# A chunked retention kernel with two matrix stages: 64-column state products, later weight splits, a second buffer and a new order of the first loads

## What is computed

```
scores = q @ k^T / 8 ; ret = scores * gamma_h^(i-j) for i >= j, else 0      8 batches, 8 heads, 576 positions, 64 wide
x  = (ret @ v), heads side by side                                          4608 tokens x 512
y  = max(x @ w1, x @ w2, x @ w3) @ w_out                                    512 -> 768 -> 512
a  = y @ u1 ; b = y @ u2 ; out = ((a * b) @ u3) @ u_out                     512 -> 1024 -> 1024 -> 512
```

## Time and profile before

| | us |
|---|---|
| median of 3 runs | 1279.63 |
| lowest, highest | 1277.74, 1281.57 |
| profiled execution | 1278.5 |
| its span in the trace | 1276.7 |
| TensorE busy | 1245.4 (98%) |
| mean granted clock of TensorE | 0.996 of 2.4 GHz |

### The profile page before, as it was taken

One profiled execution on the slowest core, in us unless ns is written; L12 is line 12 of the kernel. 1 busy time (PEld: TensorE's weight loads), 2 busy tenths in 40 slices (PEclk: granted clock), 3 DMA queues, 4 the chain that ended last, 5 costly groups with the idle time before them and its releaser, 6 DMA issues.

```text
span 1276.7 us, 20538 instructions
## 1 busy us (share of the span) xinstructions
PE 1245.4 (98%) x8032; PEld 1223.4 (96%) x8032; DVE 784.2 (61%) x1194; ACT 458.6 (36%) x707; POOL 443.0 (35%) x248
## 2 busy tenths in 40 slices
PE   7999998999999999999999999999999999799999
PEld 6999998999999999999899999999999999699998
DVE  6677755864646465559688677454545356647763
ACT  2122214432323232425455444242324234345442
POOL 4366436520202010043598571202021116525640
PEclk9999999999999999999999999999999999899999
DMA  9999865121212121043556441313223152444441
GB/s 379 309 363 298 278 212 180 62 76 49 75 50 75 50 75 44 31 138 120 180 185 213 151 145 60 106 50 100 74 94 105 51 181 83 142 155 149 155 149 69
DMA packets 82929, 174.37 MB, mean 137 GB/s; under 512 B 8976, under 2 KB 57488, under 8 KB 82832
## 3 DMA queue, kind: packets, MB, share of 16 engines
q1 hardware_dynamic: 82832, 173.05, 39.0%
HBM read 109.58 MB, written 63.44 MB: 136 GB/s over the span
## 4 chain that ended last, share of the span: by engine, by line
PE 46%; DVE 2%; issue 2%; DMA 1%; ACT 1%; SPq 0%; DVEq 0%; ACTq 0%
PE ps L965 15%; PE ps L967 15%; PE ps L966 15%; DMA gd<-h 1%; DVE clo L716 1%; DVE wlo L716 1%; ACT chi L642 0%; DVE h L804 0%; DVE h L851 0%; ACT w L706 0%; DVE h L857 0%; SPq L400 0%; DVE s L851 0%; DVE h L831 0%; DVE h L811 0%
## 5 line engine op out<-in xcount | busy, mean ns | idle before, releaser
L965 PE MATMUL ps<-chi,whi 128*128 128x384 f32 x2016 | 678.0, 336 | 20.5 <-DVE wlo L716 9.5
L966 PE MATMUL ps<-clo,whi 128*128 128x384 f32 x2016 | 676.1, 335 | 0.0
L967 PE MATMUL ps<-chi,wlo 128*128 128x384 f32 x2016 | 676.0, 335 | 0.0
L517 POOL TENSOR_TENSOR raw<-raw,raw 128x768 f32<-128x768 f32 (+2 forms) x96 | 261.4, 2743 | 594.9 <-DMA raw<-xd 207.8
L965 PEld LDWEIGHTS ps<-chi,whi 128*128 128x128 f32 x2016 | 379.7, 188 | 25.4 <-issue 11.6
L966 PEld LDWEIGHTS ps<-clo,whi 128*128 128x128 f32 x2016 | 380.0, 188 | 0.0
L967 PEld LDWEIGHTS ps<-chi,wlo 128*128 128x128 f32 x2016 | 379.8, 188 | 0.0
L716 DVE TENSOR_TENSOR clo<-raw,chi 128x768 fp32r<-128x768 f32 (+2 forms) x168 | 258.1, 1543 | 33.0 <-ACT chi L642 32.8
L642 ACT CAST chi<-raw 128x768 fp32r<-128x768 f32 (+2 forms) x168 | 180.1, 1081 | 89.7 <-PE ps L967 58.5
L706 ACT COPY w<-ps 128x384 f32<-128x384 f32 x126 | 60.5, 480 | 245.9 <-PE ps L967 244.5
L692 ACT COPY u<-ps 128x384 f32<-128x384 f32 x126 | 60.7, 481 | 169.5 <-PE ps L967 168.0
(11 more groups left out here) (41 smaller groups left out, 911.1 us busy)
## 6 DMA issues: line engine op xcount, KB each, us to landing
qks<-qk SPq DMA_DIRECT2D x32, 576.0 KB, 6.1
vks<-vk SPq DMA_DIRECT2D x32, 576.0 KB, 5.6
gd<-h SPq DMA_DIRECT2D x96, 192.0 KB, 1.9
raw<-gd SPq DMA_DIRECT2D x24, 768.0 KB, 6.4
hd<-h SPq DMA_DIRECT2D x72, 192.0 KB, 1.9
raw<-hd SPq DMA_DIRECT2D x24, 576.0 KB, 5.2
raw<-xd SPq DMA_DIRECT2D x24, 384.0 KB, 5.5
x2d<-h SPq DMA_DIRECT2D x48, 192.0 KB, 2.6
```

Of the source, the lines that this page charges most:

```text
L517: return nc.gpsimd.tensor_tensor(out_, a, b, op)
L965: nc.tensor.matmul(to, w1, x1, start=(start and k == 0), stop=False, skip_group_check=True)
L966: nc.tensor.matmul(to, w1, x2, start=False, stop=False, skip_group_check=True)
L967: last = nc.tensor.matmul(to, w2, x1, start=False, stop=(k == KH[st] - 1), skip_group_check=True)
```

## The change

It makes four edits.

- `sum_state` computes, per chunk, two products of 64 weight columns by 64 moving columns, one for each head, each into its own half of the partitions, in place of one of 128 by 128.
- Part 1 of every weight split moves: on ScalarE from after the w copy of iteration W_SPLIT_AT to before the w copy of the next iteration; on VectorE from after "21" of the next iteration to its end, just ahead of part 0 of the following weight. Weight 20, the second of stage O, is split one iteration earlier (113 in place of 114), and the first token block of stage O is split by ScalarE at the end of iteration 112 and by VectorE at the start of 113.
- In stage C a second buffer holds the block of pos 6 of every odd tile, so that its load goes out with the other three.
- The first loads go out in the order qk 0, vtab, vk 0, two heads of dec, qk 1, qtab, vk 1, the other six heads of dec.

```diff
@@ -101,13 +101,13 @@
          ("next", "p4"): [5], ("next", "p3"): [6]}
-HI_IO = {("end", "s"): [0], ("end", "u"): [1], ("end", "p3"): [2], ("end", "p2"): [3],
+HI_IO = {("prev", "w"): [0], ("end", "u"): [1], ("end", "p3"): [2], ("end", "p2"): [3],
          ("next", "p5"): [4], ("next", "p3"): [5, 6]}
...
          ("next", "12"): [5], ("next", "11"): [6]}
-LO_IO = {("end", "21"): [0], ("end", "12"): [1], ("end", "11"): [2, 3], ("next", "22"): [4],
+LO_IO = {("end", "start"): [0], ("end", "12"): [1], ("end", "11"): [2, 3], ("next", "22"): [4],
          ("next", "11"): [5, 6]}
@@ -115,6 +115,8 @@
         table = ci if tau == I * TILES else io if tau == O * TILES else std
+        if tau and it == last_of(tau - 1) - 1:
+            out += [(tau, pos) for pos in table.get(("prev", point), [])]
         if tau and it == last_of(tau - 1):
@@ -136,7 +138,7 @@
 W_SUM_AT = {2: 0, 3: 1, 4: 2, 5: 3, 6: 4, 7: 5, 8: 6, 9: 50, 10: 52, 11: 57, 12: 59, 13: 61, 14: 66, 15: 67, 16: 68,
-            17: 69, 18: 70, 19: 110, 20: 113}
+            17: 69, 18: 70, 19: 110, 20: 112}
 W_SPLIT_AT = {wi: it + (wi >= FIRST_W[C]) for wi, it in W_SUM_AT.items()}
@@ -206,13 +208,13 @@
 
-        raw_at = [[i * KH[st] * N * 4 for i in range(7)] for st in range(3)]
+        raw_at = [[i * KH[st] * N * 4 for i in range(8 if st == C else 7)] for st in range(3)]
         raw_at.append([0, 173056, 12288, 6144, 137216, 179200, 187392])
...
             kh = KH[st]
-            raw.append([at(f"raw{st}_{i}", [P, kh, N], f32, raw_at[st][i]) for i in range(7)])
+            raw.append([at(f"raw{st}_{i}", [P, kh, N], f32, raw_at[st][i]) for i in range(len(raw_at[st]))])
             size = 2 * kh * N * 4
@@ -275,7 +277,7 @@
         vk_loaded = [sem(f"vk_loaded{i}") for i in range(4)]
-        dec_loaded = sem("dec_loaded")
+        dec_loaded = [sem(f"dec_loaded{i}") for i in range(2)]
         vtab_loaded = sem("vtab_loaded")
@@ -322,6 +324,8 @@
         def raw_block(tau, pos):
+            if pos == 6 and tau // TILES == C and tau % 2:
+                return raw[C][7]
             return raw[tau // TILES][pos]
@@ -420,7 +424,7 @@
                 for pos in (0, 3, 6, 2):
-                    if pos != 6 or t == 0 or st in (B, I):
+                    if pos != 6 or t == 0 or st != O:
                         load_raw_block(tau, pos)
@@ -428,12 +432,13 @@
             load_qk(0)
-            sp.dma_start(dec[:, :, :], decay).then_inc(dec_loaded, 16)
+            sp.dma_start(vtab[:, :, :], vdecay).then_inc(vtab_loaded, 16)
             load_vk(0)
-            sp.dma_start(vtab[:, :, :], vdecay).then_inc(vtab_loaded, 16)
+            sp.dma_start(dec[:, 0:2, :], decay[:, 0:2, :]).then_inc(dec_loaded[0], 16)
+            load_qk(1)
             sp.dma_start(qtab[:, :, :], qdecay).then_inc(qtab_loaded, 16)
-            load_qk(1)
             load_vk(1)
+            sp.dma_start(dec[:, 2:HEADS, :], decay[:, 2:HEADS, :]).then_inc(dec_loaded[1], 16)
             load_u3(0)
@@ -504,7 +509,7 @@
                     load_raw(I * TILES)
-                if two_parts:
+                if two_parts and tau // TILES == O:
                     load_raw_rest(tau)
@@ -694,6 +699,9 @@
                 for wi in range(2, NW):
+                    if W_SPLIT_AT.get(wi) == it - 1:
+                        split_weight(wi, 1)
+                for wi in range(2, NW):
                     if W_SPLIT_AT.get(wi) == it:
@@ -705,9 +713,6 @@
                 splits(it, "w")
-                for wi in range(2, NW):
-                    if W_SPLIT_AT.get(wi) == it:
-                        split_weight(wi, 1)
 
@@ -718,8 +723,8 @@
                 dve.wait_ge(scored, n + 1)
-                if n == 0:
-                    dve.wait_ge(dec_loaded, 16)
+                if n < 2:
+                    dve.wait_ge(dec_loaded[n], 16)
                 if n >= 2:
@@ -737,7 +742,7 @@
                         own = slice(h * DH, h * DH + DH)
-                        new = ps[own, S_STATE, c * P + h * DH:c * P + h * DH + DH]
+                        new = ps[own, S_STATE, c * DH:(c + 1) * DH]
                         if c == 0:
@@ -817,9 +822,6 @@
                 splits(it, "21")
-                for wi in range(2, NW):
-                    if W_SPLIT_AT.get(wi) == it - 1:
-                        split_weight(wi, 1)
                 if g >= 0:
@@ -887,9 +892,12 @@
                 for c in range(NC):
-                    last = nc.tensor.matmul(ps[:, S_STATE, c * P:(c + 1) * P],
-                                            vks[n % 4][:, K_AT + c * P:K_AT + (c + 1) * P], vdec[:, c, :],
-                                            start=(c == 0), stop=(c == NC - 1), skip_group_check=True)
+                    for h in range(2):
+                        own = slice(h * DH, h * DH + DH)
+                        keys = K_AT + c * P + h * DH
+                        last = nc.tensor.matmul(ps[own, S_STATE, c * DH:(c + 1) * DH],
+                                                vks[n % 4][:, keys:keys + DH], vdec[:, c, own],
+                                                start=(c == 0), stop=(c == NC - 1), skip_group_check=True)
                 last.then_inc(state_summed, 1)
```

## The result

The changed kernel takes 1259.37 us (median of 4 runs, 1256.64 to 1261.09), the kernel before beside it 1279.14 (1277.74 to 1281.57). The ratio is 0.9841, with a 95% interval of 0.9818 to 0.9865: faster by 20 us. The forecast was 1249.4 with a range of 1243 to 1263; the sign and the range held, and the middle was 10 us too low. The profiled execution took 1258.94 us with a span of 1257.2.

What follows compares the result with a forecast made beforehand. TensorE, busy for 98% of the span, was taken to bound the kernel. 1278.5 - 16.8 - 2.0 + 0.6 + 1.5 - 2.0 - 10.4 = 1249.4 us, with a range of 1243 to 1263.

Steps and rivals of the forecast that it cites:

- State sums: First stage: eight pairs of narrow products take 0.44 us against 0.89; 0.56 us saved a step, -16.8 us over 30 steps.
- The pause: First stage: the 0.09 us pause where full-width products give way to half-width ones stays, but moves ahead of the state sum.
- The cover: First stage: with steps at 5.2 us, VectorE, GpSimd and DMA still keep up, so nothing reaches TensorE; costed at nothing.
- First loads: Start of the kernel: vtab and qk 1 land sooner, so the scores of pair 2 come at 16.3: -2.0 us (-3.5 to 0).
- Second parts, stages B and I: Later weight splits: P6's wait in B goes but sum22 comes late, +0.6 us; in I sum22 is delayed, +1.5 us.
- Second parts, stage C: Later tile changes of stage C: reordering VectorE's splits leaves their sum the same, so nothing expected (-3 to +3).
- Second buffer: Stage C, first tile change: GpSimd's chain moves up by 2.8 us, leaving 0.7 of 2.7 us of waits: -2.0 us (-3 to -1).
- Stage O: Start of stage O: 9.5 us of waits go, 1.9 come, the clock stays up saving about 4: net -10.4 us (-12 to -5).
- issue-bound sums: Rival, first stage: issue and not columns limits the sums, so 3.6 of the 16.8 us are left: 1262.6; chance 0.13.
- The stall of stage O only moves, half won: Rival, stage O: VectorE's list slips 2 us, P6 waits 2 to 3, clock falls; 6 us less won: 1255.4; chance 0.18.
- The serial halves: Rival, first stage: a sum's halves do not run side by side, sixteen products take 1.76 us: 1289.0, slower; chance 0.03.

Runs made afterwards that it cites:

- e1: The kernel before with only the state sums changed to sixteen products of 64 moving columns, loads in the old order: 1264.07 us, ratio 0.9876.
- c2: The changed kernel with the first loads back in the old order: 1256.85 us, ratio 0.9820.
- e3: The kernel before with only the second buffer for the block of pos 6 of stage C: 1273.34 us in a single run.
- e4: The kernel before with block sums of weight 20 and stage O's first token block each an iteration earlier, second parts in old places: 1270.53 us, ratio 0.9932.
- a1: The changed kernel with both engines' second weight parts back at their old places: 1254.01 us, ratio 0.9817.
- b1: a1 with sum22 ahead of the token split of pos 2 in stages C and O from the second tile on: 1249.62 us, ratio 0.9786.
- e2: The kernel before with only the second weight parts at their new places and weight 20's block sums an iteration earlier: 1275.91 us, ratio 0.997.
- a2: The changed kernel with the two loops of a state sum exchanged, halves outer: 1267.21 us in a single run.
- a3: The changed kernel with each state sum made twice, 32 products instead of 16: 1273.43 us in a single run.
- c3: The changed kernel with the first token block of stage O back at its old place: 1259.2 us (two runs).
- c4: The changed kernel without the second buffer of stage C: 1262.03 us.

## Why the prediction was right, and where it was off

- **State sums**: the mechanism was right and a size was off. I had eight pairs of 0.055 = 0.44 us; they take 0.52, which is 8 x 0.058 and an edge of 0.06 that I had removed ("the extra 0.06 at the front goes"). The pause moved to the query as forecast (+0.10) and `values` gave its 0.05. About -14.9 instead of -16.8. The cover held: in every later step nothing was late, as forecast.
- **First loads**: -2.0 forecast, nothing measured. The failed step is "pair 2 needs qk 2, whose place in the queue is unchanged ... 16.3, that is 2.4 us sooner". The place was right and the time of landing was not: qk 2 landed at 17.15, where it had landed at 16.32 in the kernel before. It landed at 16.9 to 17.7 in the eight kernels with the new order and at 15.7 to 16.5 in the six with the old; why is open. What set pair 2 before was the chain of pair 0's and 1's work, which ended 2.3 us behind that landing and which the narrow sums shorten alone (17.60 in e1, 16.28 in c2). The step ahead of it failed too: the first `vdec` was to gain 1.3 us from an earlier vtab and gained 0.6, since it also needs vk 0, which landed at 8.3 us, where it had landed at 8.2. And what is won before pair 3 is given back in the waits of the next pairs.
- **Second parts, stages B and I**: forecast +0.6 and +1.5. In B every kernel with late parts lost 1.4, and those with old ones 0 or 1.3, by whether the clock fell, mean 0.65; the difference is 0.75. Against the kernel before it is 1.4: the wait of 1.8 us went and P3 started 0.6 sooner, near the 0.7 of the forecast, but then TensorE is late not twice by 0.7 but by 0.3 to 0.6 in iterations 2, 3 and, twice, 5. In I the means are +0.2 for the six with old places (before, e1, e3, e4, a1, b1) and -1.3 for the eight with late ones, a difference of 1.5. Stage I was right; in B the mechanism was, and the size was short by 0.8 for the changed kernel.
- **Second parts, stage C**: a term that I had put at nothing. "The part 1 that leaves the chain at one place comes back at its end", so I put it down as nothing. The runs show 2.3 to 2.8 lost. Beside the second buffer 1.7 of it is waits: the weights of stage I are split there, and part 1 can now stand ahead of sum22 at a tile change (1.75 us at 674.06), where it had stood behind it. The rest is the clock, which I had not counted in this stage; without the buffer it is nearly all, and there "comes back at its end" was right for the waits.
- **Second buffer**: -2.0 forecast, -1.9 to -2.4 measured, and the number is in part luck. I had the two waits at the first tile change fall from 2.7 to 0.7 and the others stay. The w copy's 0.7 went, but sum22's 2.0 stayed in a1 and the changed kernel and fell only to 1.2 in e3; the remainder was won at a later one, the third, where the wait of 1.1 fell to 0.3 in e3 and to nothing in a1.
- **Stage O**: the waits for `wlo` went, and the clock stayed up, as forecast. Two terms were too small. Sum22 at the weight change, "about 0.4 late for P3", was 1.6 late: I had moved GpSimd's sums of weight 20 in the diff, and not laid them beside VectorE's list, where they stretch 1.75 us to 2.83. And the tile change behind, priced at 1.2, cost 1.7 to 4.5 in the seven kernels with late parts and the old order of sum22 (changed, e2, a2, a3, c2, c3, c4), 6.5 in e4's profiled execution and nothing in a1's: 2.2 of stall in the changed kernel, and 1.7 of lower clock behind it. I had counted the clock's cost for the stall that goes and not for the one that comes. Which part of the change wins the 10 us is shown in part: the second parts are not needed beside the earlier token block (e4, b1), nor the token block beside the late parts (e2, c3). What all have in common is weight 20 an iteration earlier. That edit alone was not tried.
- **Rivals**: issue-bound sums fell by a3. "The stall of stage O only moves, half won" came nearest in size, by another path than the one that I had described: not `wlo` but sum22, one tile later. The serial halves fell by every kernel with the narrow sums, and a2 shows two streams.
- **Sum of the misses**, forecast against the changed kernel's row of the table: first stage 18.8 against 15.3, B -0.6 against -1.4, C +2.0 against 0.0, I -1.5 against -0.5, O +10.4 against +6.2. That is 3.5 + 0.8 + 2.0 - 1.0 + 4.2 = 9.5 us too much; the other 0.5 of the 10.0 is the profiled executions' distance from the medians. All misses but that of stage I point the same way. The time lies outside the 1244 to 1254 to which I had given 0.61; the range held because it was drawn wide enough for the rivals.

## What to carry to other kernels

When a piece of work moves to another place in an engine's list, list every iteration in which that place occurs, with what stands behind it and what the neighbour engine does just then; the gain was in one of them and the loss in the others. Where two engines stretch each other, put the short result that TensorE waits for ahead of the long split that it needs later: one table entry won 7.5 us here. And before a microsecond or two is explained from a single pair of profiles, compare the same stretch in every trace that has the same code, and read its waits and its clock apart.

## What the runs showed of the hardware that I had not expected

- **The same stall lowers the clock in one execution and not in another.** Behind the stall of 2.1 us in iteration 1 of stage B, the kernel before ran on at the full clock and e1 did not, with the same code (length, busy PE, clock, DMA share, GB/s). The first block is of the kernel before, the second of e1. It is worth 1.3 us, and probably a part of the spread of the kernel before, 1270.79 to 1283.96 us in all its runs. At the first tile change of stage C a wait of 1.8 to 2.0 us was followed by the lower clock in seven traces and not in four (before, e1, e4, c4).

```profile
208.40:212.40 4.00, 4.00 (x23) 1.00 0.30 107
```
```profile
193.00:197.00 4.00, 3.99 (x15) 0.63 0.31 106
```

- **Column halves are two streams**, which need not alternate in the program: the next group's products start on the free half while the other still works (a2, 61.20).
- **A pause of 0.2 us stands where full-width products give way to half-width ones**, and it stays 0.2 when the last product before it has 64 moving columns and not 128 (58.16 to 58.37).
- **A load's landing moves by 2 to 3 us.** The load of pos 6 took 5.6 us in a1 and 8.8 in the changed kernel, where the loads ahead of it went out 2.0 us later, and that decided whether a stall of 2.2 us came. In b1 and e4 all four loads go out at the same points of the work, and it took 6.1 and 8.4.
